# Attention and two mixers on one core: weight pieces loaded to their low halves' places, lookahead of two, two gate buffers

## What is computed

```python
# stage 1: gated linear attention with a running state, 2 x 8 heads, 768 tokens, head width 40
m_new = maximum(f[t] + m, i[t]); f_s = exp(f[t] + m - m_new); i_s = exp(i[t] - m_new)
C = f_s * C + i_s * outer(v[t], k[t]);  n = f_s * n + i_s * k[t]
y[t] = sigmoid(o[t]) * (C @ q[t]) / maximum(abs(n @ q[t]), 1)
# stage 2: token mixing, then channel mixing
u = x + (relu(x.T @ w_tok1) @ w_tok2).T
x = u + relu(u @ w_ch1) @ w_ch2
# stage 3: real part of a 2D DFT, layer norm, channel mixing
u = x + real(fft(fft(x, axis=1), axis=2))
out = u + relu(norm(u) @ w_ch1) @ w_ch2
```

## Time and profile before

| | us |
|---|---|
| median of 3 runs | 422.52 (422.45 to 426.21) |
| the profiled execution | 419.84 |
| its span, first to last instruction | 418.0 |
| TensorE (PE) busy | 392.7 |
| VectorE (DVE) busy | 198.9 |
| ScalarE (ACT) busy | 146.2 |
| GpSimd (POOL) busy | 112.5 |
| mean granted TensorE clock | 0.971 of full |

### The profile page before, as it was taken

One profiled execution on the slowest core, in us unless ns is written; L12 is line 12 of the kernel. 1 busy time (PEld: TensorE's weight loads), 2 busy tenths in 40 slices (PEclk: granted clock), 3 DMA queues, 4 the chain that ended last, 5 costly groups with the idle time before them and its releaser, 6 DMA issues.

```text
span 418.0 us, 6305 instructions
## 1 busy us (share of the span) xinstructions
PE 392.7 (94%) x2474; PEld 374.5 (90%) x2474; DVE 198.9 (48%) x400; ACT 146.2 (35%) x317; POOL 112.5 (27%) x102
## 2 busy tenths in 40 slices
PE   8498999599799999999999999979999999999997
PEld 3387988499689999999989999969899999999997
DVE  7498573345333244214891244798855132241330
ACT  5656755444533213101360252435233032140210
POOL 5158586233723300000130049675000000000000
PEclk9869899699989999999999999999999999999999
DMA  6656577124343000000320023732000100000001
GB/s 173 195 154 194 160 214 228 48 59 158 93 127 93 19 17 0 0 17 17 110 65 31 17 76 106 209 114 96 0 2 1 49 0 17 31 2 31 17 0 49
DMA packets 18705, 31.24 MB, mean 75 GB/s; under 512 B 2628, under 2 KB 10852, under 8 KB 18676
## 3 DMA queue, kind: packets, MB, share of 16 engines
q1 hardware_dynamic: 14932, 22.94, 17.4%
q10 hardware_dynamic: 3744, 7.90, 6.6%
HBM read 26.86 MB, written 3.97 MB: 74 GB/s over the span
## 4 chain that ended last, share of the span: by engine, by line
PE 74%; DVE 6%; issue 2%; DMA 1%; SPq 1%; POOL 1%; ACT 0%; POOLq 0%; ACTq 0%
PE ps L578 28%; PE ps L557 19%; PE ps L560 3%; PE ps L559 3%; PE ps L678 3%; PE ps L458 3%; PE ps L517 3%; PE ps L434 2%; PE ps L660 2%; PE ps L535 2%; PE ps L495 2%; DVE fold L1148 2%; DMA stage<-in_ch 1%; DVE xt L1148 1%; PE ps L443 1%
## 5 line engine op out<-in xcount | busy, mean ns | idle before, releaser
L838 ACT ACTIVATE h_hi<-ps 128x384 fp32r<-128x384 f32 x88 | 43.2, 491 | 135.9 <-PE ps L560 135.9
L1090 DVE SCALAR_TENSOR_TENSOR h_lo<-ps,h_hi 128x384 fp32r<-128x384 f32 x88 | 48.8, 556 | 73.9 <-ACT h_hi L838 73.7
L1096 DVE TENSOR_TENSOR xt<-ps,xt 128x320 f32<-128x320 f32 x24 | 11.8, 491 | 78.8 <-PE ps L578 78.8
L578 PE MATMUL ps<-ch_hi,h_hi 128*128 128x320 f32 x144 | 45.4, 315 | 0.0
L578 PE MATMUL ps<-ch_hi,h_lo 128*128 128x320 f32 x144 | 44.5, 309 | 0.0
L578 PE MATMUL ps<-ch_lo,h_hi 128*128 128x320 f32 x144 | 44.5, 309 | 0.0
L458 PEld LDWEIGHTS ps<-vs,S 128*128 128x128 f32 x192 | 26.3, 205 | 14.0 <-issue 10.8
L578 PE MATMUL ps<-m_hi,h_hi 128*128 128x320 f32 x120 | 37.3, 311 | 0.0
L578 PE MATMUL ps<-m_hi,h_lo 128*128 128x320 f32 x120 | 37.1, 309 | 0.0
L578 PE MATMUL ps<-m_lo,h_hi 128*128 128x320 f32 x120 | 37.1, 309 | 0.0
L458 PE MATMUL ps<-vs,S 128*128 128x42 f32 x192 | 26.1, 289 | 11.5 <-issue 9.5
(11 more groups left out here) (153 smaller groups left out, 929.4 us busy)
## 6 DMA issues: line engine op xcount, KB each, us to landing
stage<-in_m ACTq DMA_DIRECT2D x11, 320.0 KB, 3.1
stage<-in_ch ACTq DMA_DIRECT2D x6, 384.0 KB, 4.4
vs<-in_vs SPq DMA_DIRECT2D x12, 168.0 KB, 2.7
kT<-in_kT SPq DMA_DIRECT2D x24, 80.0 KB
qz<-in_qT SPq DMA_DIRECT2D x24, 80.0 KB
og<-in_o SPq DMA_DIRECT2D x12, 160.0 KB, 3.7
ks<-in_ks SPq DMA_DIRECT2D x12, 160.0 KB, 3.4
stage<-in_ch SPq DMA_DIRECT2D x5, 384.0 KB, 4.9
```

The lines of the kernel that those rows point to most:

```text
L578: mm = pe.matmul(bank, h[hx][:, f, i * P:(i + 1) * P], w[wx][:, f], start=(f == 0 and hx == 0 and wx == 0), stop=(f == FCH[k] - 1 and hx = ...
L838: act.activation(h[0][:, f], h_bank(k, f), ACT.Relu).then_inc(hhi_done, 1)
L1090: dve.scalar_tensor_tensor(out=h[1][:, f], in0=h_bank(k, f), scalar=0.0, in1=f32(h[0][:, f]), op0=ALU.max, op1=ALU.subtract).then_inc(hlo_ ...
```

## The change

No stage buffers: each weight gets a third view of its own memory, the raw view, which lies over its low part (raw_at). A piece is loaded there, ScalarE writes the high part from it, and GpSimd subtracts in place. load_piece no longer waits; each piece has a semaphore of its own. All pieces are issued from SyncE: 0 to 3 early as before, then two with each chunk from chunk 2 on (4 and 5 with chunk 2, up to 14 with chunk 7), behind the chunk's gate input; seq and chan when the token mixing of batch 1 is done (the memory is that of tok), m1 when the last layer-1 group of block 3 is done, m2 when its last layer-2 tile is done, before x is read back. The splits of pieces are moved by one place (SPLIT_AT, SPLIT_L1): pieces are split a group later early on, and one more, 9, is split in layer 1; piece 14 goes from group 18 to 19 on GpSimd.

The gate input has two buffers, og0 and og1, each with a semaphore; load_o(1) comes before the first weight pieces, and load_o(cc) waits for gate(cc-2).

In the first batch TensorE issues log_weights(n+2) and products(n+2) ahead of in_chunk(n) (for n = 0 behind it). ScalarE does spread(1) and gate(0) in group 1, ahead of the gate sums of part 2; part 3 moves from group 4 to 5 (and 5 to 6).

```diff
-SPLIT_AT = {0: (0,), 1: (1,), 3: (2,), 5: (3,), 7: (4,), 9: (5,), 11: (6,), 13: (7,), 14: (8,), 15: (9,),
-            16: (10,), 17: (11, 12), 18: (13, 14)}
-SPLIT_L1 = {1: 10, 3: 11, 4: 12, 6: 13, 7: 14}
+SPLIT_AT = {1: (0,), 2: (1,), 5: (2,), 7: (3,), 9: (4,), 11: (5,), 13: (6,), 14: (7,), 15: (8,),
+            16: (9,), 17: (10, 11), 18: (12, 13), 19: (14,)}
+SPLIT_L1 = {1: 9, 3: 10, 4: 11, 6: 12, 7: 13, 9: 14}
-    og = at("og", o + 25728, [P, DM])
+    og = [at("og0", o + 25728, [P, DM]), at("og1", R_S, [P, DM])]
+    raw_at = {"tok1": R_T + 6144, "tok2": R_T + 18432, "ch1": R_W + 4 * 3 * F1, "ch2": R_W + 8 * 3 * F1 + 4 * 12 * DM,
+              "m1": R_W + 4 * 3 * F2, "m2": R_W + 8 * 3 * F1 + 4 * 10 * DM, "seq": R_T + 10240, "chan": o + 34048}
+    raw_flat = {n: at(f"{n}_raw", raw_at[n], [P, math.prod(two[0].shape[1:])]) for n, two in split.items()}
...
     def load_piece(eng, n):
         name, first, cols = PIECES[n]
-        before = [m for m in range(n) if slot(m) == slot(n)]
-        if before:
-            lo_split(eng, before[-1])
-        eng.dma_start(piece(n)[0], a[name][:, first:first + cols]).then_inc(ld_w[slot(n)], 16)
+        eng.dma_start(piece(n)[0], a[name][:, first:first + cols]).then_inc(ld_w[n], 16)
...
-                if cc >= 1:
-                    sp.wait_ge(eo_done, cc)
-                sp.dma_start(og[:, :], a["o"][chunk_cols(c), b * DM:(b + 1) * DM]).then_inc(ld_o, 16)
+                if cc >= 2:
+                    sp.wait_ge(eo_done, cc - 1)
+                sp.dma_start(og[cc % 2][:, :], a["o"][chunk_cols(c), b * DM:(b + 1) * DM]).then_inc(ld_o[cc % 2], 16)
...
                 load_o(cc)
-                if cc == 9:
-                    for n in range(10, 14):
-                        load_piece(sp, n)
-                if cc == 10:
-                    load_piece(sp, 14)
+                for n in range(2 * cc, min(2 * cc + 2, N_ATT)):
+                    load_piece(sp, n)
             for n in range(NT):
                 b, tile = n // NC, n % NC
+                if n == 4:
+                    sp.wait_ge(tm2_done, NT)
+                    for m in range(N_ATT, N_DFT):
+                        load_piece(sp, m)
+                if n == 9:
+                    sp.wait_ge(l1_done, FBASE[NBLK])
+                    for m in range(N_DFT, N_M1):
+                        load_piece(sp, m)
...
+            sp.wait_ge(l2_done, NT)
+            for m in range(N_M1, len(PIECES)):
+                load_piece(sp, m)
...
-            log_weights(0)
-            products(0)
+            for n in range(2):
+                log_weights(n)
+                products(n)
             for n in range(NG // 2):
                 c, g = n // 2, n % 2
-                log_weights(n + 1)
-                products(n + 1)
+                if 1 <= n <= NG // 2 - 2:
+                    log_weights(n + 2)
+                    products(n + 2)
                 if g == 1 and c >= 1:
                     from_state(c)
                 in_chunk(n)
+                if n == 0:
+                    log_weights(2)
+                    products(2)
...
-                if n == 0:
+                if n == 1:
+                    spread(1)
+                    gate(0)
                     gates_hi(2)
                 if n == 2:
                     sources_hi(2)
-                if n == 4:
+                if n == 5:
                     gates_hi(3)
-                if n == 5:
+                if n == 6:
                     sources_hi(3)
```

More of the change, by code:

```diff
@@ L1 @@
+import math
 import numpy as np
@@ L199, in build @@
     sem = nc.alloc_semaphore
-    ld_gates, ld_gates2, ld_const, ld_o = sem("ld_gates"), sem("ld_gates2"), sem("ld_const"), sem("ld_o")
+    ld_gates, ld_gates2, ld_const = sem("ld_gates"), sem("ld_gates2"), sem("ld_const")
+    ld_o = [sem("ld_o0"), sem("ld_o1")]
     ld_qk = [sem("ld_qk0"), sem("ld_qk1")]
@@ L204, in build @@
     ld_qs = [sem("ld_qs0"), sem("ld_qs1")]
-    ld_w = [sem(f"ld_w{j}") for j in range(5)]
+    ld_w = [sem(f"ld_w{n}") for n in range(len(PIECES))]
     ld_x2 = [sem("ld_x2_0"), sem("ld_x2_1")]
@@ L280, in piece @@
         hi, lo = [t[:, first:first + cols] for t in split_flat[name]]
-        return stages[slot(n)][:, 0:cols], hi, lo
+        return raw_flat[name][:, first:first + cols], hi, lo
     def loaded(eng, n):
-        eng.wait_ge(ld_w[slot(n)], 16 * sum(slot(m) == slot(n) for m in range(n + 1)))
+        eng.wait_ge(ld_w[n], 16)
     def lo_split(eng, n):
@@ L370, in _ @@
             load_kv(1)
+            load_o(1)
             load_piece(sp, 0)
@@ L428, in products @@
                     pe.wait_ge(ld_qk[t], 64 * (cc // 2 + 1))
-                if n >= NG // 2:
+                if n > NG // 2:
                     pe.wait_ge(s_done, n)
@@ L719, in split_hi @@
                 loaded(act, n)
-                if n == N_ATT:
-                    act.wait_ge(tm2_done, NT)
-                if n == N_DFT:
-                    act.wait_ge(l1_done, FBASE[NBLK])
-                if n == N_M1:
-                    act.wait_ge(l2_done, NT)
-                stage, hi, _ = piece(n)
-                act.activation(hi, stage, ACT.Copy).then_inc(whi_done, 1)
+                raw, hi, _ = piece(n)
+                act.activation(hi, raw, ACT.Copy).then_inc(whi_done, 1)
             def gates_hi(part):
@@ L792, in attend @@
                     act.activation(AB[1][64:64 + H, :], f32(g_bh[32:32 + H, :]), ACT.Copy).then_inc(ab_hi, 1)
-                if g == 0:
+                if g == 0 and cc >= 1:
                     gate(cc)
@@ L884, in _ @@
                         double(3)
-                    if k == 2 and f == 1:
-                        act.wait_ge(tm2_done, NT)
-                        for n in range(N_ATT, N_ATT + 3):
-                            load_piece(act, n)
                     if f in (4, 7, 10):
-                        n = N_ATT + 3 * (k - 2) + (f - 4) // 3
-                        split_hi(n)
-                        if n >= N_ATT + 1:
-                            load_piece(act, n + 2)
+                        split_hi(N_ATT + 3 * (k - 2) + (f - 4) // 3)
                 if k == 2:
@@ L914, in _ @@
             for n in range(N_DFT, N_M1):
-                split_more(n)
+                split_hi(n)
             for m in range(NM):
@@ L918, in _ @@
                     U_hi(0, m, half)
-                split_more(N_M1 + m)
+                split_hi(N_M1 + m)
             for n in range(N_M1 + NM, len(PIECES)):
-                split_more(n)
+                split_hi(n)
             folds_hi(1)
@@ L1325, in split_lo @@
                 pool.wait_ge(whi_done, n + 1)
-                stage, hi, lo = piece(n)
-                pool.tensor_tensor(lo, stage, f32(hi), ALU.subtract).then_inc(wlo_done, 1)
+                raw, hi, lo = piece(n)
+                pool.tensor_tensor(lo, raw, f32(hi), ALU.subtract).then_inc(wlo_done, 1)
             def attend(n):
```

21 lines of the change are left out of this document (3 added, 18 removed).

## The result

The changed kernel takes 428.75 us (median of 4 runs, 427.85 to 434.95) where the kernel before takes 422.49 us (4 runs, 419.89 to 426.21). The ratio of the two is 1.0195, with a 95% interval of 1.0119 to 1.0272. It is slower, clear of the noise, and outside my range; whether by a full 2% the interval leaves open. The profiled execution took 427.86 us with a span of 426.1, against 419.84 and 418.0 before.

What follows compares the result with a forecast made beforehand. The prediction took TensorE's own work, its gaps and the clock lost after them as the bound. Its terms summed to -5.9 us, from a median of 422.52 to 416.6, with a forecast range of 412.5 to 420 (410 to 423 with rivals).

Steps and rivals of the forecast that it cites:

- first gap: TensorE's gap at 14.4 to 20.0 us: ScalarE's new order lets weights come earlier, log_weights(6) at 32.7 instead of 36.1; -3.4 us.
- groups 6 to 12: Middle of the first attention half: ScalarE stalls TensorE, 8.4 us a chunk, but the second gap goes; +0.3 us.
- third gap: Gap at 72.1 to 78.3 us: og(7) issued near 64.5, landing in 3.4 us, so in_chunk(14) starts at 73.9; -2.0 us.
- fourth gap: Gap at 111.9 to 115.2 us: no load waits for a split any more, so SyncE no longer stands there; -5.8 us.
- wait for piece 14 and clock behind it: Layer 2: the last piece's low split moves behind the state's scaling on GpSimd; +2.1 us, and +0.9 for a lower clock.
- clock in the middle: Smaller but more frequent stalls in the middle leave one stretch of 3.4 us not covered; +1.0 us.
- late stages: Seq, chan and m pieces wait on SyncE's queue instead of being staged ahead; +0.3 us, bounds -0.3 to +1.5.
- a gap of over 2 us between 265 and 282: Sign in TensorE's late stages that would show the forecast wrong.
- my two chains: Middle: W waits behind the last chunk's finish, and og's landing delays gate, spread and W; together 8.4 us a chunk.
- Rival 2: Lookahead gives nothing net: stalls of 2 us a step, first gap's gains given back by group 12; 420.5 us, chance 0.17.
- Rival 3: Loads become the bound in the attention chunks, og landing in 6.0 us each time; 427.7 us, chance 0.08.

Runs made afterwards that it cites:

- f4: e3 with ScalarE's m2 high splits behind its first six UT_hi copies, and piece 14 split at group 18; 416.31 us, ratio 0.9907 to the kernel before.
- i1: f4 with TensorE looking one group ahead and weight pieces asked for one a chunk; 409.57 us, ratio 0.9652 to the kernel before.
- h1: e3 with ScalarE's x_hi of chunks 0 to 4 moved behind the next W, gate and spread; 418.30 us, ratio 1.0002 to the kernel before.
- h2: e3 with a chunk's og load asked for right behind its q and k; 417.95 us, ratio 0.9981 to the kernel before.
- e1: Changed kernel with its late pieces (seq, chan, m1, m2) loaded through three stage buffers as before; 422.76 us, ratio 0.9993 to the kernel before.
- e3: Changed kernel with GpSimd's five m2 low splits put behind its eo_lo splits; 420.51 us, ratio 1.0035 to the kernel before.
- f2: e3 with weight pieces 4 to 9 asked for one a chunk, 10 to 14 with chunks 8 to 10; 417.11 us, ratio 0.9876 to the kernel before.
- h3: e3 with both x_hi moved late (as h1) and og asked for early (as h2); 417.11 us, ratio 0.9946 to the kernel before.
- f3: e3 with TensorE looking one group ahead again in the first attention half; 416.67 us, ratio 0.9831 to the kernel before.
- e4: Changed kernel with ScalarE's five m2 high splits put behind its six UT_hi copies of the first batch; 423.92 us, ratio 1.0146 to the kernel before.
- e2: Kernel before with only its late pieces loaded by SyncE straight to the place of their low parts; 433.96 us, ratio 1.0366 to the kernel before.
- i2: Changed kernel with lookahead one and one piece a chunk, GpSimd's m2 low splits left as the change has them; 422.28 us, ratio 0.9968 to the kernel before.

## Why the prediction was wrong

Step by step, by the profiled runs (predicted, measured, us):

| step | predicted | measured |
|---|---|---|
| first gap, at log_weights(6) | -3.4 | -2.4 |
| groups 6 to 12 | +0.3 | +1.5 |
| groups 12 to in_chunk(14), third gap with og(7) | -1.3 | +0.4 |
| from there to log_weights(16) | 0 | -0.5 |
| fourth gap | -5.8 | -5.6 |
| wait for piece 14 and clock behind it | +2.1 +0.9 | +2.0 |
| clock in the middle | +1.0 | in the rows above |
| late stages | +0.3 | +12.6 |

**The step that failed is the late one.** I wrote: "The m2 pieces start at 266.6 and land from 270 on; ScalarE waits some 2 us for the first, between two UT_hi tiles, of which VectorE would notice 0.5." and "Term: +0.3, bounds -0.3 to +1.5." The 2 us of ScalarE were right (1.91), of which VectorE noticed 1.66. What I left out is what those pieces do once they are all there: GpSimd has five splits to do in a row, exactly beside VectorE's fold steps. I followed the loads to the engine that waits for them, and not to the engine that works on them. The trace of before had the price in it, had I looked for it: a pair of fold instructions takes 0.88 us alone, and 2.27 beside GpSimd's splits at 261 us:

```profile
260.90 2.27 DVE L1148 TENSOR_TENSOR fold<-xt 128x320 f32<-128x320 f32 x2
...
261.15 3.46 POOL L1327 TENSOR_TENSOR m_lo<-stage,m_hi 128x640 fp32r<-128x640 f32 x2 [0.32 <-ACT m_hi L727]
```

Five us of that on the way to UT_lo made a wait of 6.3, and I had no bound for a clock that falls in the late stages, since it never had. The bounds -0.3 to +1.5 were bounds of the DMA, not of the step. I had named "a gap of over 2 us between 265 and 282" as what would prove me wrong; it is there, 270.5 to 276.7.

**Right were** the fourth gap (-5.8 against -5.6, and the same in every kernel that leaves piece 14 at group 19; -4.2 in f4 and i1) and the new wait for ch_lo (2.1 against a wait of 1.74 us, and 2.0 in the stage), both worked out from what stands in a queue. The 0.9 of clock behind it did not come.

**Half right was the middle.** ScalarE's pairs of waits for og and xt came, 0.5 to 4.6 us each, and 8.4 us a chunk was 9.1. But my two chains were parts of a ring, and moving either changes nothing (h1, h2). The third gap did shrink, from 6.20 to 3.50 us, yet in_chunk(14) came only 0.5 earlier: og(7) was issued at 67.80, not 64.5, since the pace had already been lost. Rival 2 (every gain of the first gap given back, 420.5) describes the attention half best: by log_weights(14) nothing of it was left, and e1 and e3, without the late loss, can't be told from the kernel before. Rival 3 (the loads the bound, 427.7) had the right number by luck. Its waits are there, 3.5 us of TensorE for qz in four places, but og landed in 5.0 us at most, and f2, which cuts the waits for qz to 1.6 us, is no faster in the three chunks.

## What to carry to other kernels

When a change frees buffers, the work that they throttled comes in a burst: look at what the engine that consumes them runs beside, above all GpSimd splits beside VectorE instructions with two SBUF inputs, and put the burst behind the critical part in that engine's order (e3: five instructions moved, 13.7 us of the stage), after a look at what stands at the new place (h3). A term bounded by a load's landing is not yet bounded for what the data lets loose, and a gap in a stage that had none can cost more than its own length in clock (here up to 10 us behind 6.3). A deeper lookahead on one engine, with the order of the others left as it was, cost 2 us a chunk here; look at the whole ring before deepening it. Test two suspected limits together too, since one can hide the other's removal, and don't judge a variant by one trace whose time lies at the edge of its own executions (f3).

## What I had not expected of the hardware

Who pays for the contention differs from place to place. In after a fold pair of 0.89 us took 2.2 to 3.6 us, while GpSimd's splits went from 1.57 to some 1.7 us (5.06 for three): VectorE paid nearly all of it. In the kernel before, the split that began at 274.51, behind a fold step, took 1.89 us and the three together 6.54, and in e4 the first split, begun at 275.57 behind a fold step of 1.14, took 3.50: there GpSimd paid too. And an instruction with one tensor in SBUF is not safe: h3's un took 4.30 us, and e4's copy of 128x12 elements 1.42 beside a split instead of 0.18.

The clock came back later than after the earlier gaps, and not by the length of the gap. Behind the gaps of 5.6 and 6.2 us of before, TensorE worked at half clock for 8.2 and 4.5 us; behind the late gap of 6.1 to 6.3 us it did for 20.0 us in after, 17.5 in e2 and 18.4 in i2, busy all the time. e4's late gap of 2.46 us was followed by no half clock at all, h3's of 2.00 us by 6.8 us. The stretches of e2, i2 and h3 (columns as in the earlier trace rows):

```profile
285.80:303.20 17.40, 17.40 (x59) 14.43 (x59) 9.95 (x24) 2.80 (x4) 5.38 (x3) 0.50 0.16 57
...
272.60:290.90 18.30, 18.30 (x63) 15.33 (x64) 9.94 (x24) 3.14 (x5) 5.38 (x3) 0.50 0.15 54
...
291.00:297.80 6.80, 6.80 (x27) 5.90 (x25) 5.22 (x13) 1.55 (x4) 0.00 (x0) 0.50 0.00 0
```
